# Attention, spatial gating and token mixing on one core: first units re-timed, spatial rows fetched and turned sooner, last tile's products last

## The reference

```python
scores = scale * np.matmul(q, k.transpose(0, 1, 3, 2)) + bias    # -slope_h * distance
scores = np.where(is_global | is_local, scores, -1e9)
a = softmax(scores);  x = np.matmul(a, v)                         # -> [2, 768, 512]
```

```python
h = np.maximum(x @ w_in, 0.0);  u, v = h[..., :512], h[..., 512:]
v_n = (v - mean(v)) / np.sqrt(var(v) + 1e-06)
v_s = np.einsum('ts,bsd->btd', w_spatial, v_n) + b_spatial[None, :, None]
x = (u * v_s) @ w_out
```

```python
u = x + (x.transpose(0, 2, 1) @ U @ V).transpose(0, 2, 1)         # rank 32
out = u + np.maximum(u @ w_ch1, 0.0) @ w_ch2                      # 512 -> 2048 -> 512
```

## Time and profile before

| what | us |
|---|---|
| median of three runs | 538.58 |
| the three runs | 537.92, 538.58, 540.86 |
| the profiled execution | 539.94 |
| its span | 538.1 |
| PE busy in it | 521.8 (97%) |
| DVE, ACT, POOL busy | 279.3, 188.7, 132.6 |

### The profile page before, as it was taken

The page is one execution under the profiler, slowest core; times in us unless marked ns, Lnnn a source line. Parts: engine busy times, 40 slices in busy tenths (PEclk is TensorE's granted clock), DMA queues, the critical chain, the costliest instruction groups (busy, mean ns, idle before and its releaser), DMA issues.

```text
span 538.1 us, 7594 instructions
## 1 busy us (share of the span) xinstructions
PE 521.8 (97%) x2664; PEld 410.6 (76%) x2664; DVE 279.3 (52%) x769; ACT 188.7 (35%) x469; POOL 132.6 (25%) x164
## 2 busy tenths in 40 slices
PE   7799999889999999999999999999999999999996
PEld 6566666567776778888888888888888888888885
DVE  4768888876777438776424456341246523111112
ACT  3777787756657434233320010121010120101010
POOL 5843321242222001283399940000000000000000
PEclk9989999989999999999999999999999999999999
DMA  7777575656453214185033310020000002000002
GB/s 164 182 174 147 115 146 115 124 105 134 77 96 52 87 30 72 26 150 106 0 118 117 118 40 2 0 79 0 1 0 0 1 0 80 0 1 0 1 0 83
DMA packets 72010, 36.89 MB, mean 69 GB/s; under 512 B 57376, under 2 KB 66592, under 8 KB 71968
## 3 DMA queue, kind: packets, MB, share of 16 engines
q1 hardware_dynamic: 50704, 20.10, 18.2%
q0 software_dynamic: 4512, 14.29, 9.4%
q10 hardware_dynamic: 16752, 1.97, 2.7%
HBM read 32.15 MB, written 3.15 MB: 66 GB/s over the span
## 4 chain that ended last, share of the span: by engine, by line
PE 74%; DVE 3%; issue 1%; DMA 1%; ACT 1%; POOL 1%; DVEq 0%; ACTq 0%
PE ps L1407 68%; PE ps L1376 2%; PE ps L1452 1%; PE ps L1541 1%; PE ps L1424 1%; DMA wsp<-in_moe_w_spatial 1%; DVE wsp_turned L1118 1%; PE ps L1551 1%; DVE sc L1004 0%; POOL wsp L532 0%; DVE q_turned L951 0%; DVE xT_lo L977 0%; DVE gT_lo L1139 0%; DVE k_turned L951 0%; DVE pr L1019 0%
## 5 line engine op out<-in xcount | busy, mean ns | idle before, releaser
L1324 DVE SCALAR_TENSOR_TENSOR hT_lo<-ps,hT_hi 128x512 fp32r<-128x512 f32 x48 | 33.2, 692 | 167.5 <-ACT hT_hi L870 167.5
L870 ACT ACTIVATE hT_hi<-ps 128x512 fp32r<-128x512 f32 x48 | 28.7, 598 | 223.2 <-PE ps L1407 223.2
L668 ACT ACTIVATE pr<-sc,small 128x256 f32<-128x256 f32 (+1 forms) x96 | 46.3, 483 | 38.3 <-DVE small L1004 37.9
L1004 DVE CUSTOM_DVE_ANT_0 sc<-ps,bias 128x256 f32<-128x256 f32 (+1 forms) x96 | 35.0, 399 | 13.5 <-PE ps L1424 11.2
L1407 PE MATMUL ps<-win_hi,xT_hi 128*128 128x512 f32 x96 | 40.1, 418 | 0.0
L1173 DVE STREAM_TRANSPOSE ys<-tokens 32x128 f32<-32x128 f32 x128 | 38.7, 302 | 1.8
L1407 PE MATMUL ps<-win_hi,xT_lo 128*128 128x512 f32 x96 | 37.7, 393 | 0.0
L1407 PE MATMUL ps<-win_lo,xT_hi 128*128 128x512 f32 x96 | 37.5, 391 | 0.0
L1407 PE MATMUL ps<-uT_hi,w1a_hi 128*128 128x512 f32 x96 | 37.5, 390 | 0.0
L1407 PE MATMUL ps<-uT_hi,w1a_lo 128*128 128x512 f32 x96 | 37.4, 389 | 0.0
L1407 PE MATMUL ps<-w2a_hi,hT_hi 128*128 128x512 f32 x96 | 37.3, 389 | 0.0
(11 more groups left out here) (162 smaller groups left out, 1109.5 us busy)
## 6 DMA issues: line engine op xcount, KB each, us to landing
w_raw<-in_moe_w_ch POOLq DMA_DIRECT2D x16, 512.0 KB, 4.1
vn<-in_v SPq DMA_DIRECT2D x12, 256.0 KB, 3.3
out<-ys SPq DMA_DIRECT2D x12, 256.0 KB, 3.1
qk_late<-in_q SPq DMA_DIRECT2D x24, 112.0 KB, 3.8
qk_late<-in_k SPq DMA_DIRECT2D x24, 112.0 KB, 3.9
wsp<-in_moe_w_spatial POOLq DMA_DIRECT2D x28, 96.0 KB, 4.0
vp<-in_v SPq DMA_DIRECT2D x10, 224.0 KB, 4.3
w_raw<-in_moe_w_in POOLq DMA_DIRECT2D x4, 512.0 KB, 5.0
```

The lines of the kernel that those rows point to most:

```text
L668: act.activation(pr[:, k % 3, e, 0:w], sc[:, k % 2, e, 0:w], ACT.Exp, bias=nmax[:, k % 2, e:e + 1], scale=-1.0, accum_out=sums[:, k % 3, e ...
L870: act.activation(hT[0][:, n % 2, :], h1_ps(n), ACT.Relu).then_inc(s["hT_hi"], 1)
L1004: dve.tensor_tensor_reduce(out=sc[:, k % 2, e, 0:w], in0=scores_ps(k, e)[:, 0:w], in1=bias[:, 2 * p + e, WINDOW - w:WINDOW], scale=-SCALE, ...
L1324: dve.scalar_tensor_tensor(hT[1][:, n % 2, :], h1_ps(n), 0.0, hT[0][:, n % 2, :], ALU.max, ALU.subtract).then_inc(s["hT_lo"], 1)
```

## The change

Seven things are moved; no large product is added or taken away.

1. The three comparisons behind `dense_flag` and their union go from DVE to POOL (eight small operations behind its first weight transfer). DVE's patch tables are made behind `biased(1)` (`set_patches`) instead of ahead of the branch.
2. PE's second `keep_busy` of five products is gone; PE reads the flag ahead of its wait for the first keys.
3. For tile 2 the keys are fetched and turned ahead of the queries, after unit 2 and unit 3, and the queries' copy on ACT goes from unit 3 to unit 4.
4. `x_hi(0)` comes ahead of `probs_out(4)`, `x_lo(0)` ahead of `biased(7)`, and the first piece of w_in products goes from unit 6 to unit 5. Scores of unit 7 use the other PSUM banks (`FOUR = 7`) and so wait for `biased(6)`.
5. Rows 0 of `w_spatial` are fetched between chunk 4 and chunk 5, turned at unit 18 (22 before), and cast at units 19 and 23 (25 and 27 before). Rows 1 are fetched ahead of the fourth and fifth variance.
6. In the groups t, ACT's `wsp_hi` of the next rows stands ahead of `exps(a + 4)`, behind `probs_out(a + 1)`.
7. In the last two `down` steps, the products of the fourth tile come last together; the last tile is added and stored in two halves, the second on ACT's queue.

```diff
@@ gpsimd
+            pool.wait_ge(s["n_loaded"], 32)
+            for a in range(2):
+                pool.tensor_copy(flag_n[:, a:a + 1], n_raw[:, 2 * a:2 * a + 1]).then_inc(s["flag_step"], 1)
+            pool.wait_ge(s["flag_step"], 2)
+            pool.tensor_scalar(fl[:, 0:1], flag_n[:, 0:1], float(G), None, ALU.is_gt).then_inc(s["flag_step"], 1)
...
+            pool.tensor_scalar(dense_flag[:, :], fl[:, 0:1], 0.0, None, ALU.is_gt).then_inc(s["dense_ready"], 1)
...
+                if n == ready["in"]:
+                    load_rows(0, 0)
             split_u((0, 1))
-            load_rows(0, 0)
             deviation(3)
             split_u((3,))
             split_u_low()
+            load_rows(0, 1)
...
-            for t in range(1, NT):
+            for t in range(2, NT):
                 load_rows(0, t)
@@ sync
-                for a in range(2):
+                for a in (1, 0) if tile == 2 else (0, 1):
@@ scalar, unit k
-                    if k in (25, 27):
-                        wsp_hi(0, 0, (k - 25) // 2, False)
-                    if k == 3:
+                    if k in (19, 23):
+                        wsp_hi(0, 0, (k - 19) // NP, False)
+                    if k == 4:
                         set_first(2, 0, q_turned[:, 0, :, :])
+                    if k == NP:
+                        x_hi(0)
                     probs_out(k)
@@ scalar, group t
                     probs_out(a + 1)
+                    if t + 1 < NT:
+                        for h in range(2):
+                            wsp_hi(0, t + 1, h, False)
                     exps(a + 4)
                     if a + 3 <= LAST:
                         normal_half(a + 3)
-                    if t + 1 < NT:
-                        for h in range(2):
-                            wsp_hi(0, t + 1, h, False)
@@ vector, unit k
                 biased(0)
                 biased(1)
+                set_patches()
                 normalise(0)
...
-                    unit(k, False)
+                    unit(k, k == NP + 1)
...
-                    if k == 22:
+                    if k == 18:
                         turn_wsp(0, 0)
-                    if k in (25, 27):
-                        wsp_lo(0, 0, (k - 25) // 2, False)
+                    if k in (19, 23):
+                        wsp_lo(0, 0, (k - 19) // NP, False)
@@ tensor
-            pe.wait_ge(s["first_set"], 2)
-            keep_busy(0, WARM)
             pe.wait_ge(s["dense_ready"], 1)
             dense = pe.value_load(dense_flag[0:1, 0:1], min_val=0, max_val=1)
+            pe.wait_ge(s["first_set"], 2)
...
-                    unit(k, k - LAG if k >= LAG else None)
+                    unit(k, 0 if k == LAG - 1 else k - LAG if k > LAG else None)
                     if k in (2, 3):
-                        turn_first(2, k - 2)
+                        turn_first(2, 3 - k)
...
+                for tiles in (range(TB - 1), range(TB - 1, TB)):
+                    for n in (NB * NF - 2, NB * NF - 1):
+                        down(n, tiles)
```

More of the change, by code:

```diff
@@ L55 @@
 PAIRED = (ALONE + NP) // NP
-FOUR = 8
+FOUR = 7
 WARM = 5
@@ L327, in program @@
         ng, nl, gl, fl = small[:, 12:13], small[:, 13:14], small[:, 14:15], small[:, 15:18]
+        flag_n = small[:, 4:6]
         gl_win = small[:, 18:19]
@@ L468, in _ @@
                 wait(sp, "y_ready", m + 1)
-                sp.dma_start(out_d[m, :, :], ys[m % TB][:, :]).then_inc(s[f"stored{m % TB}"], 16)
+                part = slice(0, DM // 2 if m == B * NT - 1 else DM)
+                sp.dma_start(out_d[m, :, part], ys[m % TB][:, part]).then_inc(s[f"stored{m % TB}"], 16)
             for j in range(TB):
-                sp.wait_ge(s[f"stored{j}"], 16 * NB)
+                sp.wait_ge(s[f"stored{j}"], 16 * (NB + (j == TB - 1)))
         @block.gpsimd
@@ L611, in set_first @@
             def set_first(tile, a, dst):
-                act.wait_ge(s["first_turned"], 2 * tile + a + 1)
+                act.wait_ge(s["first_turned"], 6 if tile == 2 else 2 * tile + a + 1)
                 act.activation(dst, turned_first(tile, a),
@@ L683, in probs_out @@
                                probsT_ps(k)[:, :, 0:w], ACT.Copy).then_inc(s["pT_ready"], 1)
-                if k >= NP and k % NP == 0:
+                if k > NP and k % NP == 0:
                     x_hi(k // NP - 1)
@@ L882, in finish @@
                             uT_hi((n + 1) // NF, j)
+                wait(act, "y_ready", B * NT + 1)
+                act.dma_start(out_d[B * NT - 1, :, DM // 2:DM],
+                              ys[TB - 1][:, DM // 2:DM]).then_inc(s[f"stored{TB - 1}"], 16)
             with act.If(dense == 0):
@@ L958, in set_first_keys @@
             def set_first_keys(tile):
-                dve.wait_ge(s["first_turned"], 2 * tile + 2)
+                dve.wait_ge(s["first_turned"], tile + 3)
                 dve.tensor_copy(k_turned[:, :, tile, 0:P], turned_first(tile, 1))
@@ L1202, in every @@
             def every():
+                set_patches()
+                dve.wait_ge(s["iota_ready"], 7)
                 dve.wait_ge(s["bsp_loaded"], 16)
@@ L1230, in every @@
                         layer_norm(b, t)
+                        if b == 0 and t == 3:
+                            turn_wsp(0, 0)
                         if b and t < TB - 1:
@@ L1259, in turn_next @@
                         turn(k // NP + 1, q_turned[:, (k // NP + 1) % 2, :, :])
+                dve.wait_ge(s["bias_set"], 1)
                 biased(0)
                 biased(1)
+                set_patches()
                 normalise(0)
@@ L1336, in y_out @@
                     dve.wait_ge(s["uT_lo"], m + TB + 1)
-                dve.tensor_tensor(ys[j][:, :], y_ps(j), tokens[:, m, :], ALU.add).then_inc(s["y_ready"], 1)
+                parts = 2 if m == B * NT - 1 else 1
+                for a in range(parts):
+                    part = slice(a * DM // parts, (a + 1) * DM // parts)
+                    dve.tensor_tensor(ys[j][:, part], y_ps(j)[:, part], tokens[:, m, part],
+                                      ALU.add).then_inc(s["y_ready"], 1)
             def finish():
@@ L1383, in turn_first @@
                 pe.wait_ge(s["qk"[a] + qk_signal(tile)], qk_count(tile))
-                if tile == 2 and a == 0:
-                    wait(pe, "qk_turned", 2)
-                if tile == 2 and a == 1:
-                    pe.wait_ge(s["first_set"], 4)
+                if tile == 2:
+                    wait(pe, "qk_turned", 2 if a else 3)
                 for p in range(NP):
@@ L1443, in probs_v @@
                 if k == NP:
-                    wait(pe, "qk_turned", FIRST)
+                    pe.wait_ge(s["first_set"], 4)
                 if p == 0:
@@ L1566, in every @@
             def every():
-                for tile in (1, 2):
-                    for a in range(2):
-                        turn_first(tile, a)
+                for tile, a in ((1, 0), (1, 1), (2, 1), (2, 0)):
+                    turn_first(tile, a)
                 pe.wait_ge(s["first_set"], 4)
@@ L1654, in hidden, with down @@
                 ins.then_inc(s["h1_ps"], 1)
-            def down(n):
+            def down(n, tiles=range(TB)):
                 tb, f = n // NF, n % NF
@@ L1661, in down @@
                 pe.wait_ge(s["chunk_split"], ready["ch1", half] + 1 + at // 2)
-                for j in range(TB):
+                for j in tiles:
                     if f == 0 and tb:
@@ L1670, in down @@
                         ins.then_inc(s["y_done"], 1)
-                ins.then_inc(s["h2"], 1)
+                if TB - 1 in tiles:
+                    ins.then_inc(s["h2"], 1)
             def finish():
@@ L1681, in finish @@
                 down(0)
-                for n in range(1, NB * NF):
-                    if n + 1 < NB * NF:
-                        if n % NF == NF - 1:
-                            down(n)
-                            hidden(n + 1)
-                            continue
+                for n in range(1, NB * NF - 1):
+                    if n % NF == NF - 1:
+                        down(n)
                         hidden(n + 1)
+                        continue
+                    hidden(n + 1)
                     if n <= NT // 2:
@@ L1691, in finish @@
                         expand(1, 2 * n - 1)
-                    down(n)
+                    if n < NB * NF - 2:
+                        down(n)
+                for tiles in (range(TB - 1), range(TB - 1, TB)):
+                    for n in (NB * NF - 2, NB * NF - 1):
+                        down(n, tiles)
             with pe.If(dense == 0):
```

30 lines of the change are left out of this document (16 added, 14 removed).

## The result

The changed kernel took **533.82 us** (median of 4 runs, 533.47 to 534.15) against 538.99 (4 runs, 537.92 to 540.86): a ratio of 0.9897 with a 95% interval of 0.9875 to 0.992. It is faster by about 1%. The time lies in the range that was given, above the narrower band of the forecast (529.5 to 532.5) and 2.8 us above its middle of 531.0. Later comparisons ran the kernel before 43 times more, with medians of 539.99, 540.30, 539.91 and 539.69. So the three runs that the forecast started from probably lay low. Against 539.9 the gain would be 6.1 us, but the changed kernel was not run beside those 43.

What follows compares the result with a forecast made beforehand. PE was taken to carry the end, never idle from 189 us to the last product. Terms 2.9 + 0.5 + 3.2 + 0.7 + 0.3 = 7.6 us, off the median of 538.58, gave 531.0 us; range 528.8 to 534.8.

Steps and rivals of the forecast that it cites:

- narrower band of the forecast: Whole kernel: a time of 529.5 to 532.5 us, chance 0.52.
- the start gives nothing: Rival at the start: flag and branch eat the 2.4 us, or the clock falls as before; 533.9 us, chance 0.18.
- start and units: Start without the five products plus reordered units 3 to 7: 1.2 - 0.3 + 2.0 = 2.9 us gained.
- PE's new wait for x_lo(0): Unit 5, ahead of the first w_in piece: PE stands 0.7 to 0.8 us.
- no wait in group 3: Casts in the groups: PE's 0.76 us wait for a low part goes, 0.7 us gained (0.3 to 0.8).
- no PE wait over 1.5 us ahead of 100 us: Sign that the prediction holds: before 100 us PE never waits longer than 1.5 us.
- Rows 0: Earlier fetch, turn and casts of w_spatial's rows 0: 0.5 us off PE's 1.27 us wait (0 to 1.3).
- a PE wait in units 18 to 24: Sign that the prediction is wrong: PE waits in these units, where it had no wait before.
- Group 0: Earlier fetch of rows 1: project starts 2.0 us sooner, no clock fall gives 1.15; together 3.2 us (2.0 to 3.2).
- The base of the sum: The 7.6 us sum, read from an execution of 539.94 us, was taken off the median of 538.58, giving 531.0.
- the tail: Last tile added and stored in halves: 0.3 us gained, bounds -0.1 and 1.1.
- The clock rival: Units 0 to 5: PE stays at the low clock, about 9 us lost, 542.9 us, chance 0.03.

Runs made afterwards that it cites:

- e9: Changed kernel with ACT's copy of unit 26's probabilities moved ahead of unit 28's exponentials; 532.61 us, ratio to before 0.9863.
- e10: Changed kernel with the flag worked out on POOL in five operations instead of eight; 535.09 us.
- e7: Changed kernel with rows 0 of w_spatial fetched one weight chunk earlier, turned at unit 14, high and low parts both at unit 15; 534.02 us.
- e6: Changed kernel with DVE's two low parts of rows 0 one unit later (20 and 24 instead of 19 and 23); 534.38 us.
- e8: Changed kernel with the fetch of rows 1 behind the fifth variance and the first two halves of v; 534.14 us.
- e1: Changed kernel with its tail undone: last tile's products interleaved, one whole sum, one whole store on SP's queue; 533.79 us.
- e2: Changed kernel with the fetch of rows 1 of w_spatial put back behind the last tile's halves on POOL; 537.32 us.
- e3: Changed kernel with the groups' casts of w_spatial put back behind the exponential and the half scaling on ACT; 534.43 us.
- e5: Changed kernel with units 3 to 7 in the old order, FOUR 8; 535.20 us.
- e11: Changed kernel with two unread products on PE ahead of its wait for the flag; 533.35 us.

## Why the prediction held, and where it missed

**The number alone would mislead.** 533.82 us lies closer to the rival "the start gives nothing" (533.9) than to the forecast (531.0). The rows rule that rival out: start and units gave 2.88 us, as forecast. That the base of the sum and the terms that fell short add up to about the 2.9 us of that rival is chance.

**Right in mechanism and size.** The start came at 9.59 (9.5 predicted); unit 7 at 30.80 (30.5), with PE's new wait for x_lo(0) at 0.92 (0.7 to 0.8; the row names no releaser, but PE goes on 0.10 us behind x_lo's end, as it does in e9 and e10); group 0 without a DMA wait or a fall and PE's wait for the gate at 0.48 (0.4); no wait in group 3. Undone one by one they cost 0.95, 1.8, 3.5 and 0.7 us, 7.0 together, against 6.53 by which the last product came sooner. Two details differ: tile 2's queries wait 0.45 us for DVE's keys, and the flag on POOL stood at 8.43, not 8.0, its eight operations taking 2.36 us from 6.07 on. And the sign "no PE wait over 1.5 us ahead of 100 us" failed as it was worded: with nothing left to fill the time, PE stands 2.00 us ahead of the first scores.

**Rows 0, mis-sized and with the wrong cause.** The step that failed is "ahead of unit 28's bias DVE spent 0.55 on a low part at 93.72, and PE then stood 1.27 at 97.56 for the copy of unit 26. I take 0.5 off that". The stretch gained 0.02. The gap went only from 1.27 to 1.14, while a new one of 0.32 came at 81.8, in unit 23. That is one of the signs by which the prediction said it would be wrong, a PE wait in units 18 to 24. The listed waits of the stretch grew by 0.22 us; waits too small to list (0.10) and PE's busy time (68.32 to 68.18) gave it back. The low part on DVE wasn't what PE waited for: e7 took all of it away with DVE waiting for PE, and 1.07 stayed. e9 showed the releaser's own queue: the copy stood on ACT behind an exponential that waited for something else. I had read exactly that pattern for group 3 and not looked for it here, where the row names ACT's copy as the releaser.

**Group 0, right in kind and put together differently.** The 3.2 us were 2.0 of an earlier start and 1.15 of clock. Between unit 29 and 138.07 (143.85 before) PE stood idle 0.81 us instead of 2.18 and was busy 36.45 instead of 37.96, so the 2.88 are 1.37 of waiting and 1.51 of clock. The old fall lasted longer than I had read, from 116.4 to 119.8 us.

**The base of the sum.** The step "taking the same 7.6 off the median gives 531.0" took 1.36 us too much. From its own execution (539.94) the sum gives 532.3, and the profiled execution of after took 533.65; three runs of before were too few to place the median, as 43 more with a median of 539.9 suggest. Of the 2.8 us missed, 1.4 are this; the rest is rows 0 (0.5), group 0 (0.3), the tail (0.3), what lies between span and time (0.2), and the 0.2 between the profiled execution of after and its median.

**The clock rival.** "PE stays at the low clock" was given 0.03 and did not happen in the profile of after, where four unread products took 0.88 at 13.38 and 0.71 at 14.82. But it does happen, in some executions: in the profiles of e6, e8, e9 and e10 such groups of four still took 1.22 at 15.2 to 18.5 us. Its price was put at 9 us because I let it last to unit 5; it ended before 21.5 us and cost 1.6 to 3.0 us (from the first scores to unit 7 it takes 22.82 to 24.22 us instead of 21.21). The Trainium skill speaks of that ("TensorE: Matmul & The Clock Gate", Part 1): what the gate watches isn't aligned with the kernel's start, so the same kernel has different numbers of slow matmuls from run to run. The traces agree: e1, e2, e3 and e5 to e9 have the start of the changed kernel and come out in both ways, three of the eight (e6, e8, e9) slow. Whether the five products guard against it is open; the kernel before, with them, has mean clocks from 0.989 to 0.996, and its runs range over 5 us; two falls of its own are in these means.

## What to carry to other kernels

Where a row names a copy on ACT or DVE as the releaser, look at what stood ahead of that copy in its engine's queue, before blaming the engine's load: a ready step behind a wait for something else cost 0.78 us here, and one moved line gave it back. A sooner fetch that removes a wait of 2 us was worth 3.5, since the idle time of PE took the clock with it. Take a sum off the time of the execution that it was read from, and don't lean on a median of three. And when the time comes out near a rival's, go to the rows before naming the cause: here they told the two apart.

## What the runs showed of the hardware

- **Idle time ahead of a fall.** Behind the start, PE's waits of 1.63 and 1.73 (before), 1.93 (e2) and 1.96 us (e5) were each followed by a granted clock of 0.50, which began 0.15 to 2.3 us after PE had gone on; waits of 0.92, 1.14 and 1.27 us were not. At the start the length alone doesn't decide: 2.00 us (changed kernel) and 2.69 (e3) ahead of the first scores brought no fall in the reading, 2.07 (e5) and 2.12 (e11) did.
- **The granted clock and the rate differ at the start.** In the profile of e10 the granted clock reads 1.00 from 10 to 20 us while four unread products take 1.22 us, and 0.61 to 0.71 once the rate has risen. Read the duration of a known record beside it.
- **A quick beginning can turn into a slow one.** In six of fourteen profiles (e1, e5, e6, e8, e9, e11) the turn of the first tile's keys, four records near 6.5 us, ran at full rate (0.66 us) and the granted clock then fell within the idle time of 2.07 to 2.60 us ahead of the scores. In the other eight it took 1.11 or 1.12 us and the granted clock did not fall there. The fall ended by 13 us in e1, e5 and e11, and at 18.7 to 19.4 in e6, e8 and e9. Most of these kernels don't differ ahead of 7 us, so this came with the execution and not with the edit.
- **The arrival of the two numbers varies** by 0.67 us (POOL's first cast at 5.82 to 6.49), and the first scores with it (9.32 to 10.00 with the long flag).
- **Reading the flag.** From the flag's end on POOL (8.43) to the first scores (9.59) are 1.16 us, for the wait, the read into the register and the branch; it is 1.16 in e1, e3, e10 and e11 as well. The Trainium skill's 600 ns for a tensor load ("DMA: Bandwidth & Descriptors", latency and other measured facts) fits into that, and no run separates it from the branch.
- **Store landing.** The last store landed in 2.8 to 3.6 us with 128 KB on ACT's queue and 3.4 or 3.7 with 256 KB on SP's (before, e1). Stores issued 0.7 us apart don't land alike: 2.3, 3.5, 3.4 and 3.4 us in the kernel before, 2.0, 2.1 and 4.1 for the three of 256 KB in the changed one, with 2.0 for the 128 KB behind them.
